# The low part of g times the 64 remaining output channels: 64 stationary columns instead of 128, in two feed-forward layers on one core

## What is computed

```python
out = einsum('hk,bskhg->bshg', softmax(weight), x_unfolded)      # 8192 tokens x 192
h = x @ w_in                                                      # 192 -> 2048
g = where(h >= 1, h, where(h <= -1, 0, (h + 1)**2 / 4))           # layer 1
y = g @ w_out                                                     # 2048 -> 192
h = y @ w2_in ; r = maximum(h, 0) ; g = s * (r * r) + b           # layer 2
out = g @ w2_out
```

## Time and profile before

| | |
|---|---|
| median of 3 runs | 1198.95 us (1198.68 to 1199.7) |
| span of the profiled execution | 1196.3 us |
| what lies around the span, against the median | 2.65 us |
| TensorE matmuls | busy 1177.9 us (98%), 5138 instructions |
| TensorE weight loads | busy 963.1 us (81%) |
| VectorE | busy 934.8 us (78%) |
| ScalarE | busy 614.1 us (51%) |
| DMA | 17 GB/s over the span |

### The profile page before, as it was taken

How to read it: one execution, slowest core, us unless ns; L and a number is a source line. 1 busy time by engine, 2 the same in 40 slices (tenths; PEclk the granted TensorE clock), 3 DMA queues, 4 the chain that set the end, 5 groups by cost and what they waited for, 6 DMA issues and landing times.

```text
span 1196.3 us, 14126 instructions
## 1 busy us (share of the span) xinstructions
PE 1177.9 (98%) x5138; PEld 963.1 (81%) x5138; DVE 934.8 (78%) x842; ACT 614.1 (51%) x619; POOL 3.4 (0%) x16
## 2 busy tenths in 40 slices
PE   6999999999999999999999999999999999999998
PEld 3787888888888888888888888888888888888886
DVE  8999987778786877868778687787787878765555
ACT  5446654555545554545545554555545455454544
POOL 1000000000000000000000000000000000000000
PEclk9999999999999999999999999999999999999999
DMA  6003100000000000000000000001000000000000
GB/s 176 1 1 97 53 1 1 27 27 1 0 0 27 26 0 0 0 27 26 0 0 0 27 26 0 0 0 53 0 0 0 0 26 0 0 1 1 27 0 27
DMA packets 12360, 20.31 MB, mean 17 GB/s; under 512 B 1072, under 2 KB 5168, under 8 KB 12336
## 3 DMA queue, kind: packets, MB, share of 16 engines
q1 hardware_dynamic: 12256, 19.99, 5.9%
q0 software_dynamic: 64, 0.00, 0.0%
q10 hardware_dynamic: 16, 0.00, 0.0%
HBM read 13.70 MB, written 6.29 MB: 17 GB/s over the span
## 4 chain that ended last, share of the span: by engine, by line
PE 93%; DVE 5%; issue 1%; DMA 0%; SPq 0%; ACT 0%; DVEq 0%; ACTq 0%
PE h L653 46%; PE acc L666 28%; PE acc_rem L675 19%; DVE g L437 1%; DVE g_lo L455 1%; DVE mixed L489 1%; DVE mixed L503 0%; DVE mixed_rem L503 0%; DMA xraw_rem<-in_x 0%; DVE x_rem L516 0%; DVE up_lo L536 0%; DVE up_rem_lo L536 0%; DVE dn_lo L536 0%; DVE g L445 0%; DVE dn_rem L536 0%
## 5 line engine op out<-in xcount | busy, mean ns | idle before, releaser
L439 DVE SCALAR_TENSOR_TENSOR g<-r,scale,h 128x1024 f32<-128x1024 f32 x128 | 163.9, 1280 | 155.2 <-ACT r L287 154.4
L285 ACT ACTIVATE r<-h,half 128x1024 f32<-128x1024 f32 x128 | 143.1, 1118 | 272.0 <-PE h L653 264.8
L287 ACT ACTIVATE r<-h 128x1024 f32<-128x1024 f32 x128 | 131.7, 1029 | 284.9 <-PE h L653 284.3
L437 DVE TENSOR_TENSOR g<-h,r 128x1024 f32<-128x1024 f32 x128 | 156.6, 1223 | 93.3 <-ACT r L285 92.7
L458 DVE SCALAR_TENSOR_TENSOR g_lo<-g,shift,g_hi 128x1024 fp32r<-128x1024 f32 x128 | 163.7, 1279 | 0.0
L666 PE MATMUL acc<-g_hi,dn_hi 128*128 128x512 f32 x512 | 160.0, 394 | 3.1 <-DVE g_lo L455 1.6
L653 PE MATMUL h<-x_hi,up_hi 128*128 128x512 f32 x512 | 157.9, 390 | 3.0 <-DVE g L437 1.7
L653 PE MATMUL h<-x_rem,up_rem_hi 128*128 128x512 f32 x512 | 157.9, 390 | 2.5 <-DVE x_rem L516 2.5
L675 PE MATMUL acc_rem<-g_lo,dn_rem 128*128 128x512 f32 x512 | 157.9, 389 | 0.0
L675 PE MATMUL acc_rem<-g_hi,dn_rem 128*128 128x512 f32 x512 | 157.9, 389 | 0.0
L666 PE MATMUL acc<-g_lo,dn_hi 128*128 128x512 f32 x512 | 157.9, 390 | 0.0
(11 more groups left out here) (87 smaller groups left out, 963.3 us busy)
## 6 DMA issues: line engine op xcount, KB each, us to landing
xraw<-in_x SPq DMA_DIRECT2D x7, 518.0 KB, 4.4
out<-res SPq DMA_DIRECT2D x7, 512.0 KB, 3.3
stage<-in_moe_w_out SPq DMA_DIRECT2D x6, 384.0 KB, 3.4
xraw_rem<-in_x SPq DMA_DIRECT2D x14, 129.5 KB, 4.0
out<-res_rem SPq DMA_DIRECT2D x7, 256.0 KB, 3.6
stage<-in_moe_w_in SPq DMA_DIRECT2D x2, 512.0 KB, 5.2
stage<-in_moe_w_in SPq DMA_DIRECT2D x4, 256.0 KB, 5.2
xraw<-in_x SPq DMA_DIRECT2D x1, 512.0 KB, 4.2
```

The costliest lines, as they stand in the source:

```text
L285: nc.scalar.activation(r[k][:], h[k][:], ACT.Relu, scale=0.5, bias=half[:, 0:1]).then_inc(r_ready, 1)
L287: nc.scalar.activation(r[k][:], h[k][:], ACT.Relu).then_inc(r_ready, 1)
L437: nc.vector.tensor_tensor(g[k][:], h[k][:], r[k][:], ALU.max).then_inc(h_used, 1)
L439: nc.vector.scalar_tensor_tensor(g[k][:], r[k][:], scale[:, 0:1], h[k][:], ALU.mult, ALU.mult).then_inc(h_used, 1)
```

## The change

In each step's `down`, the pass of line 675 that has g_lo as its moving operand takes only the high weights as its stationary operand: `dn_rem[layer][:, j, 0, :]`, 64 columns, and it writes only the rows 0 to 63 of `acc_rem`. The product of the low weights and g_lo, which the rows 64 to 127 also gathered, is no longer computed. In a phase's last chunk (j = 15) the two passes change places, so that the accumulation ends with a matmul on all 128 rows; `rem_summed` goes with it. The number of matmuls, their moving operands and every wait stay.

```diff
-                w = dn_rem[layer][:, j].rearrange("p a d -> p (a d)")
-                order = [(n, t) for n in range(2) for t in range(B)]
+                both = dn_rem[layer][:, j].rearrange("p a d -> p (a d)")
+                parts = [(both, g_hi, acc_rem), (dn_rem[layer][:, j, 0, :], g_lo, acc_rem[0:REM])]
+                end = j == CH - 1
+                order = [(n, t) for n in ((1, 0) if end else (0, 1)) for t in range(B)]
                 for n, t in (sorted(order, key=lambda nt: nt[1]) if final else order):
-                    last = nc.tensor.matmul(acc_rem[:, t, :], w, (g_hi, g_lo)[n][k][:, t, :],
-                                            start=(j == 0 and n == 0), stop=(j == CH - 1 and n == 1))
-                    if final and n == 1:
+                    w, v, dst = parts[n]
+                    last = nc.tensor.matmul(dst[:, t, :], w, v[k][:, t, :],
+                                            start=(j == 0 and n == 0), stop=(end and n == 0))
+                    if final and n == 0:
                         last.then_inc(rem_summed, 1)
```

## The result

The changed kernel takes 1206.06 us (median of 4 runs, 1205.62 to 1206.14) against 1199.09 us for the kernel before (4 runs, 1198.68 to 1199.7): ratio 1.0058, 95% interval 1.0043 to 1.0072. I had forecast no change, 1198.9, in a range that ended at 1201.0.

The account below looks back on a forecast made before the run. The prediction took TensorE's time from one matmul to the next, 226.7 ns, as the bound. All terms were 0 against the profiled span of 1196.3 us; the runs' median lies 2.65 us above, giving 1198.9, range 1192 to 1201.

Parts of the forecast that it names:

- the 13.3 ns: Each matmul's start to start of 226.7 ns beyond 213.3 ns of streaming 512 columns; width's share taken as 0.
- Narrower loads: 512 matmuls load 64 columns: record near 0.133 us, 28 us less PEld busy time, hidden with 0.1 us to spare, so 0.
- The row that I misread: Kernel start: pair before a late load's matmul took 0.47 us, as did a pair with timely loads; claimed 0.1 us to spare.
- rival 2: Slower: changing stationary width between 128 and 64, twice a step, 512 changes, stops the array; chance 0.14.
- small form: Rival 2 with another 13.3 ns at each width change: 6.8 us, 1205.7; chance 0.06 for a few ns per change.
- large forms: Rival 2 with the array running empty: 0.087 us per change, 44.5 us, 1243.5; upper bound 83 us, 1282; chance 0.08.
- Rival 1: Faster: the load's width is in the 13.3 ns; half saved gives 1195.5, all gives 1192.1; chance 0.24.
- The exchange of the passes: The two passes change places in 16 of 256 steps, the same four matmuls run: 0.

Follow-up runs that it names:

- e2: Changed kernel with 64 stationary columns in nearly every matmul of the steps, leaving out half the hidden channels and much of the output: 1212.75 us, ratio 1.0117.
- e3: Changed kernel with line 678's four matmuls sorted by half t in every step, so narrow and wide alternate: 1203.09 us, ratio 1.0034.
- e8: Changed kernel with 124 stationary columns in the g_lo pass of every step instead of 64: 1199.03 us, ratio 1.0003.
- e10: Changed kernel with 88 stationary columns in the g_lo pass of every step instead of 64: 1198.82 us, ratio 0.9999.
- e1: Changed kernel with the narrowing undone and the exchange of the two passes in each phase's last chunk kept: 1198.64 us, ratio 1.0.

## Why the prediction was wrong

- **"The whole question is whether the 13.3 ns belong to the width of the weights."** That was the wrong question. The narrow load gives nothing (e2: 230 ns a matmul with every load narrow), as I said. But I had read 226.7 ns as a price per matmul that can be added up, and it is the settled state of a rhythm, which can be lost.
- **"Narrower loads ... On the path it is worth nothing if the load is hidden ... I take 0."** This term failed. Hidden it was, down to the forecast record (133 against 134 ns) and 27 us of PEld time (28), and it had 0.1 us to spare. The spare time is there in the trace after as well: a narrow load ends 93 ns before its matmul starts (median). It cost 33 ns a step all the same, 7.3 us in the sum: 12 ns in the narrow pair (236 + 229 against 453) and the other two thirds in the wide matmuls behind it, which my sum didn't contain.
- **The row that I misread.** To show that a late load does no harm I compared 0.47 us after a wait with 0.47 us of another pair of the same stretch, and took both as normal. Both were high against the steady 0.453 (469 and 463 ns from the trace's starts): they were settling. So that row couldn't show that the matmul wasn't some ns late. The right reading was a restart that costs the next matmuls several ns each without any wait, and the question what else would set it off. The restart that I did price, 0.087 us in rival 2, is one of the two that settle at once, so it showed nothing of such a stretch.
- **Rival 2 had the sign, and its small form had 1205.7.** That is within 0.4 us of the result, but by a price of 13.3 ns at each of 512 changes of width, and the runs took this mechanism away: twice the changes cost less (e3), 124 and 88 columns cost nothing (e8, e10). So the number was luck: a right number from a wrong mechanism. I gave that form 0.06 and cut the range at 1201.0 right before it, because no row showed a change of width; that a case isn't in the trace was a reason for a wider range, not for a lower chance. Its large forms (1243.5 and 1282) didn't occur: there is no idle time at a change. The Trainium skill's rule in "TensorEngine Tiling (Array Packing)", Key Properties, that a change of tiling mode drains the TensorE, shows no effect here (PE idle 0.0 us before the narrow pass); its "PSUM — Partial Sum Buffer", The four PSUM rules, by which float32r takes the full column group anyway, agrees with that.
- **Rival 1** fell with e2. The rule of the Trainium skill's "Trainium Kernel Development and Optimization", Performance Expectations, that the share of LDWEIGHTS tells how near the roofline is, doesn't serve here: from 963.1 us of PEld to 704 us the kernel became 1.2% slower.
- **The rest held.** The exchange of the passes costs nothing (e1), no wait grew, the matmul records of the wide passes that are not in the settling stretch stay at 389 ns, and the clock stayed full.

## What to carry to other kernels

In this kernel, where TensorE streams nearly without a pause, the time from one matmul to the next is a settled rhythm, and an edit to one matmul had to be priced over some ten behind it. Where a kernel looks the same, compare starts to the nanosecond, group by group, also of the passes that the edit doesn't touch. Less work in a hidden operation isn't free of risk: where columns were saved in an operand whose loads are hidden anyway, no run here won anything, and up to 60 ns an occurrence were lost. A sweep of the disturbance over the steps of one run gives a whole table of prices, and it forecast four kernels to 0.1%.

## What the runs showed of the hardware that I had not expected

- A stream of float32r matmuls of 128 x 512 settles at 226.7 ns from start to start; with 64 stationary columns in all of them it is 230.0 ns, slower, with a cycle of six: 234, 230, 236, 229, 224, 227.
- After a wait, a narrower matmul or a shorter stream, the next 3 to 11 matmuls mostly go through a sequence that often ends in 236, 228, 232, 231, 227 ns. The kernel before pays it at 26 of the 28 places where it leaves the rhythm. Pairs of 124 and 88 stationary columns and of 510, 496, 480, 464 and 416 moving ones set nothing off.
- The price has no order in the size of the disturbance: 0 ns for 124 and for 88 columns, 60 ns for a pair of 120, 40 ns for a pair that streams 508 columns instead of 512.
- A load's record goes evenly with its columns in the kernels run whole: 188, 184, 181, 161 and 134 ns for 128, 124, 120, 96 and 64.
